# Low parts of late weight pieces on GpSimd, and an earlier split of the next x half, in a token mixer

## The reference, cut to what matters

```python
def _moe_ref(x, w_theta, w_tok_r, w_tok_i, w_ch):        # x: 4 x 768 x 384
    theta = x @ w_theta
    zr = x * cos(theta)
    zi = x * sin(theta)
    y = einsum('ts,bsd->btd', w_tok_r, zr) + einsum('ts,bsd->btd', w_tok_i, zi)
    u = x + y
    return u + maximum(u @ w_ch, 0.0)
```

## Time and profile before

| what | us |
|---|---|
| median of 3 runs | 640.92 |
| the profiled execution | 640.71 |
| its span, first to last instruction | 639.0 |
| TensorE matmul busy in the span | 594.3 |
| TensorE weight load busy | 571.2 |
| VectorE busy | 367.5 |
| ScalarE busy | 290.2 |
| GpSimd busy | 35.8 |

### The profile page before, as it was taken

How to read it: one execution, slowest core, us unless ns; L and a number is a source line. 1 busy time by engine, 2 the same in 40 slices (tenths; PEclk the granted TensorE clock), 3 DMA queues, 4 the chain that set the end, 5 groups by cost and what they waited for, 6 DMA issues and landing times. The chain is left out here.

```text
span 639.0 us, 12023 instructions
## 1 busy us (share of the span) xinstructions
PE 594.3 (93%) x4262; PEld 571.2 (89%) x4262; DVE 367.5 (58%) x618; ACT 290.2 (45%) x513; POOL 35.8 (6%) x68
## 2 busy tenths in 40 slices
PE   1998999479989999999999989999999999999998
PEld 1888888379889999999999987998999899989998
DVE  7899997157769444844664354676425632562141
ACT  5799996345555333522542224633431343144112
POOL 2233332000000000000000000000000000000000
PEclk9999999779979999999999989999999999999999
DMA  7879987480321023023000514430021002000102
GB/s 191 203 221 253 252 243 236 134 263 0 92 95 38 25 75 95 34 70 95 16 21 30 173 63 132 138 115 0 2 82 68 0 0 74 0 0 14 63 0 75
DMA packets 32411, 58.77 MB, mean 92 GB/s; under 512 B 3824, under 2 KB 24304, under 8 KB 32368
## 3 DMA queue, kind: packets, MB, share of 16 engines
q1 hardware_dynamic: 32368, 58.21, 30.3%
HBM read 44.04 MB, written 14.16 MB: 91 GB/s over the span
## 5 line engine op out<-in xcount | busy, mean ns | idle before, releaser
L997 PE MATMUL mix_ps<-w_hi,z_hi 128*128 128x384 f32 x288 | 99.7, 346 | 2.5 <-DVE z_lo L77 2.5
L997 PE MATMUL mix_ps<-w_lo,z_hi 128*128 128x384 f32 x288 | 97.7, 339 | 0.0
L997 PE MATMUL mix_ps<-w_hi,z_lo 128*128 128x384 f32 x288 | 97.6, 339 | 0.0
L997 PE MATMUL gate_ps<-w_hi,w_lo 128*128 128x384 f32 x192 | 64.2, 334 | 0.0
L997 PE MATMUL gate_ps<-w_hi 128*128 128x384 f32 x192 | 64.1, 334 | 0.0
L997 PE MATMUL gate_ps<-w_lo,w_hi 128*128 128x384 f32 x192 | 64.1, 334 | 0.0
L997 PEld LDWEIGHTS mix_ps<-w_hi,z_hi 128*128 128x128 f32 x288 | 54.6, 190 | 3.7 <-issue 3.7
L997 PEld LDWEIGHTS mix_ps<-w_lo,z_hi 128*128 128x128 f32 x288 | 54.5, 189 | 0.0
L997 PEld LDWEIGHTS mix_ps<-w_hi,z_lo 128*128 128x128 f32 x288 | 54.4, 189 | 0.0
L72 ACT ACTIVATE g_hi<-gate 128x384 fp32r<-128x384 f32 x32 | 16.8, 526 | 76.1 <-DVE gate L1873 76.1
L1869 DVE TENSOR_TENSOR gate<-gate_ps,b_all 128x384 f32<-128x384 f32 x32 | 17.8, 556 | 56.9 <-PE gate_ps L997 56.5
(11 more groups left out here) (129 smaller groups left out, 1387.5 us busy)
## 6 DMA issues: line engine op xcount, KB each, us to landing
f_raw<-in_fT_dram SPq DMA_DIRECT2D x32, 144.0 KB, 3.7
k_raw<-in_kT_dram SPq DMA_DIRECT2D x32, 144.0 KB, 3.1
q_raw<-in_qT_dram SPq DMA_DIRECT2D x32, 144.0 KB, 3.6
v_raw<-in_vC_dram SPq DMA_DIRECT2D x16, 288.0 KB, 4.1
xT<-y_sb SPq DMA_DIRECT2D x32, 144.0 KB, 3.5
w_raw<-in_wB_dram SPq DMA_DIRECT2D x6, 768.0 KB, 6.5
xt<-xT SPq DMA_DIRECT2D x8, 576.0 KB, 4.1
u<-xT SPq DMA_DIRECT2D x8, 576.0 KB, 5.4
```

The source lines that it names most:

```text
L997: done = pe.matmul(out, a, b, start=(first and n == 0), stop=(last and n == len(terms) - 1))
```

## The change

Weight pieces 2 to 6 get their low part from GpSimd (a tensor_tensor subtract of the same shape) and no longer from VectorE. mix(2,0) to mix(5,0) and channel(0) wait for GpSimd's semaphore. Pieces 0 and 1 stay with VectorE. `x_hi(0)` and `x_lo(0)` move up by one mixing step. In the attention, two semaphores counted by VectorE become one with the sums 2, 4 and 5; the same instructions wait for the same VectorE memsets.

```diff
+        wlo_done = sems.enter_context(nc.semaphore("b_wlo_done"))
...
         @block.gpsimd
+            for n in range(2, ST + 1):
+                pool.wait_ge(wb_hi, n + 2)
+                pool.tensor_tensor(w_lo[:, weights(n)], w_raw[:, weights(n)], w_hi[:, weights(n)].bitcast(F32), ALU.subtract)\
+                    .then_inc(wlo_done, 1)
...
         @block.scalar
-                (z_up(3), 1), (to_turns(4), 1), (trigs(4), 1), (xn_out(5), 1), (weights_up(4), 1), (w_in_up(2), 1), (w_in_up(3), 1),
-                (z_up(4), 1), (to_turns(5), 1), (trigs(5), 1), (x_hi(0), 0), (xn_out(0), 0), (weights_up(5), 1), (w_in_up(4), 1),
+                (z_up(3), 1), (to_turns(4), 1), (trigs(4), 1), (xn_out(5), 1), (x_hi(0), 0), (weights_up(4), 1), (w_in_up(2), 1), (w_in_up(3), 1),
+                (z_up(4), 1), (to_turns(5), 1), (trigs(5), 1), (xn_out(0), 0), (weights_up(5), 1), (w_in_up(4), 1),
...
         @block.tensor
-                        pe.wait_ge(wb_lo, s + 2)
+                        if s < 2:
+                            pe.wait_ge(wb_lo, s + 2)
+                        else:
+                            pe.wait_ge(wlo_done, s - 1)
...
-                    if first(b) and g == 0:
-                        pe.wait_ge(wb_lo, ST + 2)
+                    if g == 0:
+                        pe.wait_ge(wlo_done, ST - 1)
...
         @block.vector
-                (weights_down(0), 0), (z_down(1), 1), (reduce(2), 1), (u_down(0), 2), (u_down(1), 2), (x2_down, 2), (multiply(2), 1), (weights_down(2), 1),
+                (weights_down(0), 0), (z_down(1), 1), (reduce(2), 1), (u_down(0), 2), (u_down(1), 2), (x2_down, 2), (multiply(2), 1),
                 (z_down(2), 1), (reduce(3), 1), (add_channel(0), 2), (multiply(3), 1), (add_channel(1), 2),
-                (weights_down(3), 1), (w_in_down(0), 1), (w_in_down(1), 1),
-                (z_down(3), 1), (reduce(4), 1), (add_channel(2), 2), (multiply(4), 1), (add_channel(3), 2),
-                (weights_down(4), 1), (w_in_down(2), 1), (w_in_down(3), 1),
-                (z_down(4), 1), (reduce(5), 1), (add_channel(4), 2), (multiply(5), 1), (x_lo(0), 0), (add_channel(5), 2), (weights_down(5), 1), (w_in_down(4), 1),
+                (w_in_down(0), 1), (w_in_down(1), 1),
+                (z_down(3), 1), (reduce(4), 1), (add_channel(2), 2), (multiply(4), 1), (add_channel(3), 2), (x_lo(0), 0),
+                (w_in_down(2), 1), (w_in_down(3), 1),
+                (z_down(4), 1), (reduce(5), 1), (add_channel(4), 2), (multiply(5), 1), (add_channel(5), 2), (w_in_down(4), 1),
...
-                (add_mix(3), 1), (x_lo(1), 0), (weights_down(1), 0), (add_mix(4), 1), (add_mix(5), 1), (weights_down(6), 1)], 2)
+                (add_mix(3), 1), (x_lo(1), 0), (weights_down(1), 0), (add_mix(4), 1), (add_mix(5), 1)], 2)
```

More of the change, by code:

```diff
@@ L181, in attention @@
         cleared = {name: sems.enter_context(nc.semaphore(f"{name}_cleared")) for name in "fqk"}
-        y_cleared = sems.enter_context(nc.semaphore("y_cleared"))
-        carry_cleared = sems.enter_context(nc.semaphore("carry_cleared"))
+        rest_cleared = sems.enter_context(nc.semaphore("rest_cleared"))
+        Y_CLEARED, ENDS_CLEARED, KV_CLEARED = 2, 4, 5
         cap_set = sems.enter_context(nc.semaphore("cap_set"))
@@ L325, in chunk_ends @@
                 if first(p):
-                    act.wait_ge(carry_cleared, 2)
+                    act.wait_ge(rest_cleared, ENDS_CLEARED)
                 act.wait_ge(st_sb.h, st_sb.at(p.back(2), 1))
@@ L408, in states @@
                 if first(p):
-                    pe.wait_ge(carry_cleared, 3)
+                    pe.wait_ge(rest_cleared, KV_CLEARED)
                 pe.wait_ge(st_sb.h, st_sb.at(p.back(1), 1))
@@ L427, in f @@
                     if first(p):
-                        pe.wait_ge(y_cleared, 2)
+                        pe.wait_ge(rest_cleared, Y_CLEARED)
                     pe.wait_ge(y_sbd.h, y_sbd.at(p.back(1), half + 1))
@@ L475, in _ @@
             for half in range(2):
-                dve.memset(y_ps_[half][32:64, 0:384], 0.0).then_inc(y_cleared, 1)
+                dve.memset(y_ps_[half][32:64, 0:384], 0.0).then_inc(rest_cleared, 1)
             for i in range(2):
-                dve.memset(ends[i][:, :], 0.0).then_inc(carry_cleared, 1)
-            dve.memset(kv_ps_[:, 0:NCHUNK * HDIM], 0.0).then_inc(carry_cleared, 1)
+                dve.memset(ends[i][:, :], 0.0).then_inc(rest_cleared, 1)
+            dve.memset(kv_ps_[:, 0:NCHUNK * HDIM], 0.0).then_inc(rest_cleared, 1)
             def keep_in_range(p, b):
```

## The result

The changed kernel takes 648.9 us, the median of 4 runs (647.05 to 652.29); the kernel before 641.33 us over 4 runs beside them. The ratio is 1.0125, with a 95% interval of 1.0075 to 1.0175: slower by 1.25%, about 8 us.

A forecast was written before the change was run, and what follows sets the result against it. TensorE's matmuls fill 93% of the span, fed in the first batch by the nearly as tight z loop. Loop delay 5.8 plus clock 2.4 gave 8.2 us on 640.7, 648.9, median 649.1; 8-in-10 range 641.0 to 652.5.

The forecast's parts named there:

- GpSimd's price: One late piece's subtraction of 1536 columns on GpSimd, a form not in the trace: taken at 3.5 us.
- The port: SBUF reading, seen in the attention: GpSimd reads and VectorE instructions with two SBUF inputs exclude each other; VectorE held 0.32 us.
- Only one row shows VectorE held up: Point granted to the rival "the port is no obstacle", about the attention's row of 1.27 us where 0.95 was usual.
- The walk: First batch's z loop timed step by step with GpSimd's piece in it: second batch's mix(0,0) 5.8 us later.
- Part 2: x_hi(0) and x_lo(0) one step up: the stall at 178.40 and its half clock disappear, but the gain stops at mix(0,0).
- The clock: Lowered TensorE clock for the 3.2 us wait at the loop's end, ahead of the second batch's mix(0,0): +2.4 us.
- The sum: Whole kernel: 5.8 + 2.4 = 8.2 us on the profiled 640.7, 648.9; median of the runs 0.2 above, 649.1.
- the port is no obstacle: Rival: GpSimd's reading doesn't hold VectorE's subtractions; second batch's mix(0,0) 5.2 us earlier, about 636 us; chance 0.16.
- rival of a quick piece: GpSimd's piece takes 1.6 us; second batch's mix(0,0) 1.8 us earlier, clock takes 2.6: 641.5, no change; chance 0.10.
- the 6.2 us at theta(0): TensorE's 3.56 us stall for x_lo(0) ahead of the next batch's theta, with 2.6 us lost to half clock.

The follow-up runs named there:

- write-only: The changed kernel, but GpSimd fills each late low piece with zeros in two memsets in place of the subtraction; 0.9955 of the kernel before.
- the copying kernel: The changed kernel, but GpSimd copies w_hi into w_lo (one input) in place of the subtraction; 0.9971 of the kernel before.
- the move alone: The kernel before with only x_hi(0) and x_lo(0) moved up, all weight pieces on VectorE; 0.9993 of the kernel before.
- the other execution of before's mixer: The kernel before with only the attention's two semaphores merged, its mixer unedited; 0.9993 of the kernel before.
- the quarters: The changed kernel, but GpSimd makes each late piece in instructions of 384 columns, four for 1536; 1.0074 of the kernel before.
- the new tail order: Kernel before, x halves moved up, add_mix(0) and add_mix(1) ahead of reduce(1), last w_in part's split behind z(0); 0.9965.
- the gap kernel: The new tail order, with late pieces 2 to 5 split in ScalarE's and VectorE's idle time; 0.9916 of the kernel before, again 0.9912.

## Why the prediction was right

The forecast was 649.1 us, the result 648.9. By its steps, each distance counted from z_lo(1)'s end:

- *GpSimd's price.* Taken at 3.5 us from the masks' rate, between 2.9 and 4.2; the rows show 3.49 for the free ones. The estimate of 3.4 us from the Trainium skill, "GPSIMD Engine Reference", section "Performance versus the Vector engine", was 0.1 us low.
- *The port.* Read from one row of 1.27 us in place of 0.95 and one of 2.32. The change shows it at full size, and the write-only and the copying kernel show that the reading does it. "Only one row shows VectorE held up" was a misreading: in the trace of before a second ks, at 25.64, took 1.27 us as well, beside two masks. The rule of the Trainium skill, "SBUF — State Buffer", section "Who interferes with whom", names also a second conflict: instructions such as tensor_scalar, when they run in one of VectorE's two-port modes, contend with GpSimd. I used only the half of it that the trace of before showed, and the write-only run missed its expectation in good part by that; there the tensor_scalar of 1.45 us agrees with the second half.
- *The walk.* Later by 1.3 us at mix(2,0), 3.5 at mix(3,0), 6.2 at mix(4,0) and 5.4 at the next mix(0,0), where the text had 1.35, 3.6, 6.5 and 5.8. As distances from z_lo(1)'s end they are 9.7, 20.2, 31.8 and 53.9 us for 9.8, 20.4, 32.0 and 54.3; these don't hang on which execution of before is taken, while against the other one mix(0,0) is later by 6.5 us and not 5.4. The waits at the last three: 2.07, 3.09 and 3.64 us for 2.3, 3.4 and 3.2. At mix(5,0) the text had no wait and 2.6 us of half clock instead; there was no half clock, and a wait of 1.60 us. Either fits into the room ahead of the next mix(0,0), so the sum didn't notice. Piece 6 held z_lo(1) of the second batch by 1.55 us (2.50 for 0.95), as the text had it, and TensorE's next wait, 0.36 us at turn(4), was no longer than in before.
- *Part 2.* The stall at theta(0) went and the gain stopped at mix(0,0), shown by the move alone.
- *The clock.* Taken at 2.4 us. The 3.7 us at 0.54 behind the last wait cost 1.7 us, and the shorter wait at turn(4) gave 0.3 back. B grew by 6.7 us and A by 5.4, so 1.3 us came in behind mix(0,0). This is the term that was mis-sized most, nearly twice what came.
- *The sum.* 5.4 + 1.3 = 6.7 us in the profile against 8.2 forecast; the runs gave 7.6 us between medians, with an interval of 4.8 to 11.2. Against the other execution of before's mixer B grew by 6.8 us, so the sum is firm and its split between loop and clock isn't. That 649.1 and 648.9 lie so close is luck: the profile's sum is 1.5 us below the forecast, and medians of the kernel before moved by 2 us between sessions.

The rival "the port is no obstacle" fell with the first long z_lo. The rival of a quick piece is borne out as a mechanism by the copy, but its time was some 2.5 us too high (641.5, where 0.9971 of 640.9 is 639.0), mainly because it charged for a half clock that didn't come.

## What to carry to other kernels

Work that is moved to GpSimd isn't off VectorE if GpSimd reads SBUF and VectorE's own instructions next to it have two SBUF inputs: the piece then stays on the chain at GpSimd's length, here twice VectorE's, and no row calls it a wait; look for VectorE rows that have grown. A tensor_scalar was held even by a memset. Before work is moved to another engine, look for the gap in the same engine's chain (here 1.58 us a step, during the sines). And a stall removed from the bounding engine is worth no more than the slack up to its next supplier: the 6.2 us at theta(0) were worth nothing while the loop behind them was long, and with the loop shortened they went without moving x_lo. Last, hold an edit's effect in one trace against two traces of an unedited kernel: here such a pair lay 1.1 us apart.

## What I hadn't expected of the hardware

- A write-only GpSimd memset held a tensor_scalar (1.45 us in place of 0.36) and not a tensor_tensor with two SBUF inputs (0.96 us) that ran beside it.
- The clock doesn't follow from a wait's length alone. Waits of 1.60, 2.03, 2.07, 2.33, 3.03 (mix(4,0) with the quarters) and 3.09 us left it at full speed. Those of 1.92 us (turn(4) with the pieces alone on GpSimd: mean clock 0.61 over the next 4 us), 2.06 us (mix(4,0) there: 0.62 over 3.5 us), 2.20 us (semaphores merged), 3.02, 3.56, 3.64, 3.70 and 4.37 us were followed by half clock.
- Even one and the same wait goes both ways. The 2.08 us for u_lo in the last batch stand in all twelve traces; in seven the mean clock over the next 5 us is 0.66 (before, the change, the x halves alone, the pieces alone, the new tail order, the gap kernel twice), in the other five 1.00. What decides stays open; no run was made on it.
- Instructions of 384 columns on GpSimd against VectorE alternate, one and one: the rows of one step end at 161.82 (GpSimd), 162.24 (VectorE), 163.11, 163.52, 164.40, 165.21, 166.07 and 166.28. This keeps every single delay under 1 us and still costs: 4.8 us lost in place of 8.
